# Attention inside an MLP kernel: causal blocks of 64 by 64 tokens, a state in the middle of the chunk, and three places per chunk instead of two

## The reference

```python
state = alpha[:, :, t, :, None] * state + np.einsum('bhd,bhe->bhde', k[:, :, t], v[:, :, t])
y[:, :, t] = np.einsum('bhd,bhde->bhe', q[:, :, t], state)      # for t in range(768)
...
xn = (x - mu) / np.sqrt(var + 1e-06) * g_ln                     # first MLP
x = x + np.maximum(xn @ w_ch1, 0.0) @ w_ch2
...
u = x + real(fft(fft(x, axis=1), axis=2))                       # second MLP
out = u + np.maximum(norm(u) @ w_ch1, 0.0) @ w_ch2
```

## Time and profile before

| | |
|---|---|
| median of 3 runs | 792.5 us (792.22 to 798.42) |
| the profiled execution: time, and span of its instructions | 792.46 us, 791.0 us |
| TensorE busy | 782.1 us, 99% |
| VectorE, ScalarE, GpSimd busy | 468.0, 214.5, 55.3 us |
| attention under the MLPs | about 36 to 390 us of the span |

### The profile page before, as it was taken

One profiled execution on the slowest core, in us unless ns is written; L12 is line 12 of the kernel. 1 busy time (PEld: TensorE's weight loads), 2 busy tenths in 40 slices (PEclk: granted clock), 3 DMA queues, 4 the chain that ended last, 5 costly groups with the idle time before them and its releaser, 6 DMA issues.

```text
span 791.0 us, 13706 instructions
## 1 busy us (share of the span) xinstructions
PE 782.1 (99%) x5426; PEld 765.2 (97%) x5426; DVE 468.0 (59%) x1049; ACT 214.5 (27%) x424; POOL 55.3 (7%) x109
## 2 busy tenths in 40 slices
PE   8999999999999999999999999999999999999998
PEld 7998999999999999999999999999999999999998
DVE  7988585856667476577486775437543564342422
ACT  3543232232312322223234333112221232111211
POOL 1000000000000000000001300210012000300000
PEclk9999999999999999999999999999999999999999
DMA  9343113031130420431323511120002100000000
GB/s 253 120 139 88 49 56 112 31 106 62 37 99 31 107 70 31 126 106 45 130 71 100 180 70 51 41 101 31 1 31 86 45 0 18 12 1 31 0 31 31
DMA packets 29814, 53.89 MB, mean 68 GB/s; under 512 B 1916, under 2 KB 24700, under 8 KB 29756
## 3 DMA queue, kind: packets, MB, share of 16 engines
q1 hardware_dynamic: 29756, 53.10, 21.4%
HBM read 43.65 MB, written 13.37 MB: 72 GB/s over the span
## 4 chain that ended last, share of the span: by engine, by line
PE 86%; issue 6%; DVE 5%; ACT 1%; POOL 1%; DMA 0%; POOLq 0%; DVEq 0%
PE h L95 12%; PE acc L97 12%; PE acc L95 12%; PE acc L96 12%; PE h L97 11%; PE h L96 11%; PE side_bank L1393 4%; PE side_bank L1349 2%; PE side_bank L1383 2%; PE side_bank L1401 2%; PE side_bank L96 2%; PE side_bank L97 2%; PE side_bank L95 1%; PE side_bank L1363 1%; PE side_bank L1333 1%
## 5 line engine op out<-in xcount | busy, mean ns | idle before, releaser
L169 DVE SCALAR_TENSOR_TENSOR hT_low<-h,hT_high 128x384 fp32r<-128x384 f32 (+1 forms) x204 | 108.5, 532 | 178.7 <-ACT hT_high L164 178.0
L95 PE MATMUL h<-xnT_high,w_high 128*128 128x384 f32 (+1 forms) x612 | 205.4, 336 | 1.4 <-DVE hT_low L169 1.4
L97 PE MATMUL h<-xnT_high,w_low 128*128 128x384 f32 (+1 forms) x612 | 199.4, 326 | 0.0
L96 PE MATMUL h<-xnT_low,w_high 128*128 128x384 f32 (+1 forms) x612 | 199.3, 326 | 0.0
L95 PE MATMUL acc<-w_high,hT_high 128*128 128x384 f32 x576 | 194.0, 337 | 0.0
L164 ACT ACTIVATE hT_high<-h 128x384 fp32r<-128x384 f32 (+1 forms) x204 | 96.3, 472 | 359.4 <-PE h L97 359.2
L97 PE MATMUL acc<-w_high,hT_low 128*128 128x384 f32 x576 | 192.9, 335 | 0.0
L96 PE MATMUL acc<-w_low,hT_high 128*128 128x384 f32 x576 | 192.5, 334 | 0.0
L95 PEld LDWEIGHTS h<-xnT_high,w_high 128*128 128x128 f32 x612 | 115.2, 188 | 5.0 <-DVE hT_low L169 1.7
L96 PEld LDWEIGHTS h<-xnT_low,w_high 128*128 128x128 f32 x612 | 115.3, 188 | 0.0
L97 PEld LDWEIGHTS h<-xnT_high,w_low 128*128 128x128 f32 x612 | 115.0, 188 | 0.0
(11 more groups left out here) (123 smaller groups left out, 768.6 us busy)
## 6 DMA issues: line engine op xcount, KB each, us to landing
stage<-w_dram SPq DMA_DIRECT2D x24, 384.0 KB, 3.6
x_scratch<-x_unit SPq DMA_DIRECT2D x8, 576.0 KB, 3.3
a_in<-alpha_dram SPq DMA_DIRECT2D x6, 672.0 KB, 5.1
q_in<-q_dram SPq DMA_DIRECT2D x6, 672.0 KB, 7.5
k_in<-k_dram SPq DMA_DIRECT2D x6, 672.0 KB, 8.7
v_in<-v_dram SPq DMA_DIRECT2D x6, 576.0 KB, 3.8
xb<-x_scratch SPq DMA_DIRECT2D x4, 576.0 KB, 4.2
xb<-x_turned SPq DMA_DIRECT2D x4, 576.0 KB, 6.8
```

Source lines behind the costliest of these rows:

```text
L95: pe.matmul(out, wh, xh, start=start, stop=False)
L96: pe.matmul(out, wh, xl, start=False, stop=False)
L97: return pe.matmul(out, wl, xh, start=False, stop=stop)
L169: dve.scalar_tensor_tensor(out=self.hT[1][:, j % H_SLOTS, 0:u.cols], in0=self.hps[j % H_BANKS][:, 0:u.cols], scalar=0.0, in1=self.hT[0][:, ...
```

## The change

Each chunk is treated as two halves of 64 tokens (`SUBS`), and a chunk takes three slots.

- `scores`: only the two diagonal blocks of 64 keys by 64 queries are computed, 16 matmuls, each on one quarter of the array (64 rows by 64 columns). `probs` halves to 128x256, `causal` to a 64-wide triangle in both halves of the partitions.
- `increments`: one per half, 16 matmuls with 64 keys each. The first half's go to `bank[BKU]`, the second half's to `second_bank`, which is `bank[BY]`; so they wait until the masks have read the scores. The last chunk now has transposes and the first half's increments too.
- `next_state` first writes a middle state (state before plus first half, `MIDDLE`), then the state after. The first chunk of a sequence does the same additions.
- `outputs_within`: 16 matmuls of `probs` and `v_in`, 64 by 64, on two diagonal quarters of the array. `outputs_carried`: 8 matmuls (4 for the first chunk), 112 rows by 64 columns: queries of the first half read the state before, those of the second half the middle state.
- In units of three chunks the slots are scores 0, 3, 6; increments and within 1, 4, 7; carried 2, 5, 8. VectorE now prepares q and k of a slot before the mask of that slot.
- In the first unit, `first_increments` uses all 128 keys for the second bank, and ScalarE writes the middle state.

```diff
-        self.scores, self.outputs = (1, 4, 7), (2, 5, 8)
-        self.q_slots, self.k_slots = {0: 1, 3: 2}, {2: 1, 4: 2}
-        self.next_slot, self.next_k_slot, self.rows_slot, self.range_slot = 7, 7, 9, 4
+        self.scores, self.within, self.carried = (0, 3, 6), (1, 4, 7), (2, 5, 8)
+        self.q_slots, self.k_slots = {3: 2}, {2: 1, 5: 2}
+        self.next_slot, self.next_k_slot, self.next_q_slot = 6, 8, 10
...
-ONE[1].scores, ONE[1].outputs, ONE[1].range_slot = (5, 8), (6, 9), 7
-ONE[2].scores, ONE[2].outputs = (3, 5), (4, 6)
+ONE[1].scores, ONE[1].within, ONE[1].carried, ONE[1].range_slot = (4, 8), (5, 9), (6, 9), 7
+ONE[2].scores, ONE[2].within, ONE[2].carried = (3, 6), (4, 7), (5, 8)
...
+ONE[2].next_q_slot, ONE[3].q_slots = None, {1: 1, 3: 2}
...
             def next_state(u, c):
...
+                dve.wait_ge(u_summed, g + 1)
+                dve.wait_ge(s_ready, g + 1)
+                for two, rows in enumerate(HR):
+                    op = dve.tensor_tensor(middle[rows, :, two, :], added(bank[BKU], rows), held[rows, :, two, :], ALU.add)
+                op.then_inc(half_ready, 1)
...
                 for two, rows in enumerate(HR):
-                    op = dve.tensor_tensor(state_sum[rows, :, :], added(rows), held[rows, :, two, :], ALU.add)
+                    op = dve.tensor_tensor(state_sum[rows, :, :], added(second_bank(u), rows), middle[rows, :, two, :],
+                                           ALU.add)
...
                 for h in range(PAIRS):
-                    for two in range(2):
-                        op = pe.matmul(score_bank(u, two)[:, h * P:(h + 1) * P], k_div[HR[two], s, h, :],
-                                       q_mul[HR[two], s, h, :], start=True, stop=True)
+                    for sub in SUBS:
+                        for two in range(2):
+                            op = pe.matmul(score_bank(u, two)[sub, h * SUB:(h + 1) * SUB], k_div[HR[two], s, h, sub],
+                                           q_mul[HR[two], s, h, sub], start=True, stop=True)
...
+            def increment(psum, c, h, two, rows):
+                head = 2 * h + two
+                return pe.matmul(psum[HR[two], h * D:(h + 1) * D], k_divT[rows, h, HR[two]],
+                                 v_in[rows, c, head * D:(head + 1) * D], start=True, stop=True)
...
+            def increments(u, c):
...
+                    pe.wait_ge(sc_masked, 2 * g + 2)
+                for h in range(PAIRS):
+                    for psum, rows in zip((bank[BKU], second_bank(u)), SUBS[:1] if u.last(c) else SUBS):
+                        for two in range(2):
+                            op = increment(psum, u.slot(c), h, two, rows)
...
+            def outputs_within(u, c):
...
                 for h in range(PAIRS):
                     for two in range(2):
...
+                        for i, sub in enumerate(SUBS):
+                            pe.matmul(y[sub, cols], probs[two][sub, h, :], v_in[sub, s, cols],
+                                      start=h == two == 0, stop=u.new(c) and i == 0 and h == PAIRS - 1 and two == 1)
+
+            def outputs_carried(u, c):
+                s, g, y = u.slot(c), u.base + c, y_bank(u)
+                pe.wait_ge(half_ready, g + 1)
+                for h in range(PAIRS):
+                    for i, sub in enumerate(SUBS):
+                        if i == 0 and u.new(c):
+                            continue
+                        op = pe.matmul(y[sub, h * 2 * D:(h + 1) * 2 * D], q_mul[:, s, h, sub],
+                                       state[:, (u.state_slot(c), MIDDLE)[i], h, :, :].rearrange("p two e -> p (two e)"),
+                                       start=False, stop=h == PAIRS - 1)
```

More of the change, by code:

```diff
@@ L781, in side_one @@
                 for c in range(u.size):
-                    if slot == u.scores[c] and not u.last(c):
+                    if slot == u.scores[c]:
                         copy_kT(u, c)
-                    if slot == u.outputs[c]:
+                    if slot == u.carried[c]:
                         copy_y(u, c)
@@ L996, in mask @@
                     dve.tensor_tensor(probs[two][:, :, :],
-                                      score_bank(u, two)[:, :].rearrange("p (h t) -> p h t", h=PAIRS),
-                                      causal[:, None, :].to_broadcast([P, PAIRS, P]), ALU.mult).then_inc(sc_masked, 1)
-            def next_state(u, c):
-                if u.last(c):
[L1002 to L1015, removed]
-                        op = dve.tensor_tensor(to[rows, :, two, :], added(rows), decay(rows), ALU.mult)
-                    op.then_inc(u_read, 1)
-                    dve.wait_ge(u_read, done)
+                                      score_bank(u, two)[:, 0:PAIRS * SUB].rearrange("p (h t) -> p h t", h=PAIRS),
@@ new lines, in next_state @@
+            def next_state(u, c):
+                g = u.base + c
+                held, middle = state[:, u.state_slot(c), :, :, :], state[:, MIDDLE, :, :, :]
+                to = state[:, u.state_slot(c + 1), :, :, :]
+                dve.wait_ge(u_summed, g + 1)
+                dve.wait_ge(s_ready, g + 1)
+                for two, rows in enumerate(HR):
+                    op = dve.tensor_tensor(middle[rows, :, two, :], added(bank[BKU], rows), held[rows, :, two, :], ALU.add)
+                op.then_inc(half_ready, 1)
+                dve.wait_ge(half_ready, g + 1)
+                if u.last(c):
+                    dve.sem_inc(u_read, 1)
@@ L1360, in increments @@
+            def outputs_within(u, c):
+                s, g, y = u.slot(c), u.base + c, y_bank(u)
+                wait_v(u, c)
+                pe.wait_ge(sc_masked, 2 * g + 2)
+                if u.first() and c > 0:
+                    pe.wait_ge(x_ready, g)
                 for h in range(PAIRS):
                     for two in range(2):
-                        head = 2 * h + two
-                        op = pe.matmul(bank[BKU][HR[two], h * D:(h + 1) * D], k_divT[:, h, HR[two]],
-                                       v_in[:, s, head * D:(head + 1) * D], start=True, stop=True)
@@ L1411, in side_one @@
                     if slot == u.scores[c]:
-                        if not u.last(c):
-                            transpose_k(u, c)
+                        transpose_k(u, c)
                         scores(u, c)
-                    if slot == u.outputs[c]:
-                        if not u.last(c):
-                            increments(u, c)
-                        outputs(u, c)
+                    if slot == u.within[c]:
+                        increments(u, c)
+                        outputs_within(u, c)
+                    if slot == u.carried[c]:
+                        outputs_carried(u, c)
                 for k in TRANSPOSES_ONE.get(slot, ()):
```

161 lines of the change are left out of this document (95 added, 66 removed).

## The result

| | before | after |
|---|---|---|
| median | 792.43 us (8 runs) | 786.54 us (8 runs, 786.5 to 788.0) |
| ratio, 95% interval | | 0.9912 (0.9885 to 0.9940) |
| span of the profiled execution | 791.0 us | 785.0 us |
| first MLP matmul of the program starts at | 25.02 us | 31.79 us |

The change makes the kernel faster by 5.9 us, 0.7% of the median. Forecast were 15.7. Two of the eight runs of the kernel before took some 6 us more than the other six (such runs show a mean granted clock of 0.989 to 0.991, the others 1.00); the median hardly feels them, while the ratio, here and in the experiments, counts them in and so comes out lower than the medians' own quotient, 0.993.

What follows compares the result with a forecast made beforehand. TensorE, busy for 782 of 791 us, was taken as the bound. Jobs -19.3, the start -1.0 and waits for VectorE +4.6 made -15.7, so 776.8 us, range 768 to 790.

Steps and rivals of the forecast that it cites:

- The jobs: TensorE's three jobs per chunk: transposes and scores 1.20, increments and within 1.63, carried 1.02 us; -19.3 us over 22 chunks.
- Issue-bound passes: Rival, 18%: small passes issue only every 0.0225 us, so scores and increments each take 0.72; +12.0, 788.8 us.
- One bank, one row half: Rival, 6%: row halves writing one bank in `outputs_within` cannot overlap; within takes 1.87, second job 2.57; 796 us.
- Row halves stop overlapping: Rival, 7%: with columns cut too, all three 64x64 jobs lose row overlap, first job costing 1.67 again; 812 us.
- VectorE late in steady units: Rival, 9%: TensorE meets one wait of 0.75 us in ten places there; +7.5, 784 us.
- The start: First unit's chain: two masks shorter by 0.53 each, middle addition beside the outputs; -1.0 us, bounds 0 and -1.5.
- Behind a waiting TensorE instruction stands the whole MLP: Sentence on new waits: increments wait for both masks, carried for the middle state; a steady unit's slots were walked.
- VectorE late: TensorE's waits for k_div, probs and xn_one before 145 us, in two-chunk units' short slots; +4.6 us, bounds 0 and 8.
- the wait of 0.80 before `normalise`, which was to go: Term of the waits for VectorE: one wait of 0.8 us near 136 us disappears.
- The sum is about zero: VectorE's work per chunk: mask -0.53 against middle state's two instructions, 0.70; hidden in steady units.
- The closing test: Whole kernel: a total above 785 us with jobs at their sizes would mean VectorE's slack was misread.

Runs made afterwards that it cites:

- run 10: Changed kernel with the loop over a chunk's halves outermost in `scores`, so neighbouring matmuls stand on two quarters of the array, not four; 792.2 us, single run.
- run 9: Changed kernel with the loop over the halves outermost in `outputs_within`, so 16 neighbouring passes use the same quarter of the array; 802.04 us, single run.
- Run 1: Changed kernel with the first unit's identity-matmul (`keep_clock`) arguments back to 2, 2, 0, 9 instead of 10, 9, 4, 26; 782.97 us.
- run 2: Changed kernel with only the first unit's last block of identity matmuls cut from 26 to 9; 783.89 us.
- run 3: Kernel before, attention untouched, with identity-matmul arguments raised to 10, 13 and 26 instead of 2, 2 and 9; 799.09 us.
- run 5: Changed kernel, first unit reordered: second chunk's transposes and scores ahead of `outputs_carried(0)`, keys copied ahead of first output, identity counts 10 and 10; 781.73 us.
- The best version: Number 8: on run 7, one unit's carried job a slot later, and queries, keys and scores moved so the middle state is ready in time; 777.94 us.
- run 7: On top of run 5, scores one slot later in units whose keys came late, some carried jobs moved too; 779.99 us.
- Run 6: Changed kernel with VectorE lightened: a chunk's eight scans (F and F_inv) replaced by two plain copies; 778.36 us, single run.
- run 4: Changed kernel with no identity matmuls at the four places of the first unit (0, 0, 0, 0); 784.92 us.

## Why the prediction was right and wrong

*The jobs: right.* Forecast 1.20, 1.63 and 1.02 us, measured 1.21, 1.64 and 1.01, so -19.3 us stands. Four quarters run together (run 10 takes that away), two diagonal ones do too (run 9), and the carried job goes at the pace of its moving columns, 0.083 a step, not of its 64 loaded ones.

*Issue-bound passes: fell.* 32 passes of the increments take 0.39 us from their first start to that of within, 0.012 each. The Trainium skill, TensorE: Matmul & The Clock Gate, section "Wait — 56ns, not 53.3ns?", has 25 ns as the least from start to start; with passes on different quarters the trace shows half of that, and the measurement decides.

*One bank, one row half: fell.* The second job costs 1.64 and not 2.57, although both row halves write the output's bank, in different partitions. The restriction of TensorEngine Tiling (Array Packing) in the Trainium skill, section Restrictions and Gotchas, is therefore not what this trace shows for such halves.

*Row halves stop overlapping: fell* with the first job, 1.21 and not 1.67. *VectorE late in steady units: fell*; from 150 to 400 us TensorE waits for none of it.

*The start: wrong, and the step that failed.* "Two masks are shorter by 0.53 each and the middle addition lies beside the outputs: -1.0 us". Measured +6.8, 7.8 us off and outside both bounds. I followed VectorE's chain and did not count what the diff puts on TensorE itself: 72 identity passes more, and `outputs_carried(0)` with its new wait for VectorE's signal of the middle state ahead of the next chunk's transposes. The prediction's sentence "Behind a waiting TensorE instruction stands the whole MLP" was applied to the steady units and not to the start. Run 1 gives 3.5 us to the counts, 3.1 of which run 2 finds in the last block alone; run 3 finds 6.7 by the counts alone in the kernel before; run 5 gives 0.9 us of MLP start more to the order. The best version still starts 1.9 us later than before (26.92), with the clock at half for a part of it (0.66 from 11 to 16 us); but run 7, at full clock in its profile, starts at 26.93 too. TensorE pauses there for 1.30 us in the increments (the view calls it issue), and behind that stands VectorE, by run 7's timeline:

```profile
19.64 0.72 DVE L1047 TENSOR_TENSOR state<-side_bank,state 48x192 f32<-48x192 f32 x2 [1.58 <-PE acc L1403]
20.39 0.72 DVE L1055 TENSOR_TENSOR state_sum<-acc,state 48x192 f32<-48x192 f32 x2
21.15 0.72 DVE L1060 TENSOR_TENSOR state<-state_sum,F 48x192 f32<-48x192 f32 x2
21.90 0.56 DVE L1064 BATCH_NORM_STATS2 stats<-x_unit 128x6 f32<-128x384 f32 x1
```

So the other half of the step was wrong too: the middle addition does not lie beside the outputs but in series: it takes 0.75 us ahead of both state steps and the statistics; before, two state steps stood there (18.93 and 19.69, statistics at 20.44). With the pause of 1.30 us, for which the trace names no cause, that is about the 1.9 us. No run takes either of them away, so what holds this last part of the start is read from one trace and not shown.

*VectorE late: right in place and kind, too small.* Forecast +4.6 at k_div, probs and xn_one before 145 us (its terms add up to 4.5), measured +6.3 (bounds 0 and 8), the last at 149 us. Run 6 shows the cause. Place by place: the first MLP's keys 0.71 (forecast 0.7), sequence 1's first chunk 1.07 (1.0), its second 1.68 (1.2), the next unit's first 1.51 (1.1); and the wait of 0.80 before `normalise`, which was to go, is there again at 141 us. These last three are 1.7 us of the difference. "The sum is about zero" for VectorE's own work was a little short: by its own terms it is 0.70 - 0.53 = 0.17 a chunk, 4 us over 24 chunks, and VectorE is busy 472.0 us instead of 468.0.

So the total missed by 9.8 us: 7.8 from the start and 1.7 from the waits; 0.3 is what the three sums leave open. The closing test, that a total above 785 with jobs at their sizes would mean misread slack of VectorE, named the smaller of the two causes only.

## What to carry to other kernels

Small matmuls whose loads and outputs lie on different 64x64 quarters of the array start together, and the innermost loop must walk over the quarters for it: a step then costs nearly the same for one, two or four of them (0.052 to 0.059 us here). When a change shortens TensorE's part, reckon the fill-in matmuls and the order of the start anew, since they are the part of the path that no steady unit shows; count them in the diff like any other work. Look also for where a signal is given: here TensorE could take up a state that was ready at 12.74 us only at 16.27. A wait that goes from one slot to the next is only gained if the engine that is waited for has idle time there.

## What the runs showed that I had not expected

- 64 by 64 passes alone on a quarter follow each other after 0.052 us (run 9), in four quarters after 0.012 to 0.015 each.
- Passes of another quarter begin ahead of their turn: in run 10 the second half's scores start beside the first half's, and the first increments before the last scores.
- The granted clock fell to 0.5 for over 3 us at about 17 us after a wait of 1.8 us (run 1), at 16.6 and at 23.4 us after waits of 2.2 and 2.4 (run 4), and not where the wait was 0.80 (after) or 0.47 (run 2). Runs 3, 5 and 8 show a fall at 12.14, 11.95 and 12.07 us. Ahead of it TensorE had waited 0.80, 1.03 and 0.98 us for the first chunk's keys, in runs 3 and 5 another 0.51 and 0.59 for their copy, and the 44 identity passes of the opening, the same in all kernels, had ended sooner than in the others (6.66 to 6.75 us long; 6.77 to 7.90 elsewhere). Run 9, with a wait of 0.92 us there, has no fall, and run 7, with run 5's start, has neither the wait nor the fall: it differs from execution to execution, and what decides it I cannot say.
- Fewer identity passes at the four places gain first and then no more: medians of 786.5 us with 98, 783.9 with 64, 783.0 with 26, 784.9 with none, where the last two differ by less than the scatter of their runs.
